# Attention sums of two neighbouring chunks issued as one stretch of array tiles

## The chip, the cores and the metric

The kernel runs on one core of one Trainium2 chip. The metric is the device time of one execution in microseconds (us), the lower the better. PE is the matrix engine (TensorE), PEld its weight loads, DVE the vector engine, ACT the scalar engine, POOL the general engine, SP the engine whose queue issues most of the DMAs. SBUF is the on-chip memory and PSUM the eight banks that matrix products are written to.

## What is computed

Three layers follow each other. The first is a linear attention with a decaying state, for 4 batches, 8 heads, 768 tokens and head dimension 48; the second a dense layer pair with a sigmoid-gated activation (3072 tokens, 384 to 2048 to 384); the third a soft mixture of 8 experts with 32 slots.

```python
for t in range(S):                                  # attention
    cur = np.einsum('bhd,bhe->bhde', u[None] * kt, vt)
    y[:, :, t] = np.einsum('bhd,bhde->bhe', rt, state + cur)
    state = wt[:, :, :, None] * state + np.einsum('bhd,bhe->bhde', kt, vt)
h = x @ w_in                                        # dense pair
x = (h * (1.0 / (1.0 + np.exp(-1.702 * h)))) @ w_out
logits = x @ phi                                    # soft experts
slot_input = softmax over tokens (logits).T @ x
out = softmax over slots (logits) @ expert outputs
```

## The kernel before

**Chunks and steps.** The tokens are cut into 24 chunks of 128 (six to a batch), and the chunks into 9 steps of 2, 2, 2, 3, 3, 3, 3, 3 and 3 chunks (`SIZES`, `BASE`). The dense pair works on a step at a time. Its hidden dimension of 2048 is cut into 16 parts, so there are 9 x 16 = 144 numbered slots `F`, with `i, f = divmod(F, 16)`. In slot F, PE issues the 9 hidden products of part F (L1272, bank `hps[F % 2]`, 256 or 384 tokens wide) and then the products of the second matrix for part F - 2 (L1407, three for each chunk of its step). ACT makes the activation (L804) and its rounded copy `gh` (L808), which waits for the second-matrix products that PE issues in the same slot, and DVE the remainder `gl` (L1111).

**The order is written out by hand.** The list `slots_of_work` says which further work stands in which slot, and each engine's program walks through the same list; each executes its own instructions strictly in this order, with semaphore waits between the engines. While step i is in the dense pair, the attention of the chunks of step i + 1 is made, in four parts `j` for each chunk (`hosts`: in a step of three chunks slots 0 to 3, 4 to 7 and 8 to 11), and behind them the expert logits of step i - 1 (`gather`).

**The attention of a chunk**, for 4 pairs `p` of heads (`par` is the head of a pair, rows 0 to 47 or 64 to 111) and its two halves `c` of 64 tokens:
- DVE scans the decays forward (`decays`, L915) and backward (`invert`, L934 and L938), makes the decayed r (`decayed`, `rp`, L944), the grown keys (`grown_keys`, `kd`, L949) and the bonus products `ruk` (L922). These are made for chunk n + 1 in the slots of chunk n, as `front_part`.
- j = 0: PE makes the scores (L1205, banks `zps`, `yps`), and turns the keys (L1306, bank `mps`), which ACT copies to `kn` (L761); DVE masks the scores (L974).
- j = 1: PE sums the bonus over each head (L1427, L1429, into `mps`), DVE multiplies it by v into `ybuf` (`bonus_values`, L985, counted by `uv_done`).
- j = 2: PE makes the state sums (L1216: keys times values of each half, into `zps` and `yps`), DVE the states `midway`, `grown` and `state` (L994, L1000, L1007).
- j = 3: PE makes the outputs (`output`, L1225 from the states, L1231 from the masked scores, into `zps` and `yps`), DVE adds them to `ybuf` (L1017). SP stores it to a scratch tensor, and loads it again as `x` in the layout of the dense pair; ACT and DVE split it (`splits`, L417, L503).

Scores, state sums and outputs are products of 48 or 64 rows by 48 or 64 columns. They run in quarters of the array: the quarter is given by the half of the rows that is read and the half of the rows that is written. The output products from the states read and write the same half, so they use two of the four quarters; the others use all four. One product of float32 operands is two records in the trace. All of `mps` is shared: key turns, bonus sums, turns of x (L1481), logits (L1494) and others are written there in turn, and before each PE waits for the reader of the last one (`mps_read`).

**Weights.** The two weight matrices are cut into quarters, eight pieces in all, that ACT rounds (`high_at`, L741) and DVE subtracts (`low_at`, L1083) in slots of step 0; the hidden products of F = 4, 8 and 12 and the second-matrix products of parts 0, 4, 8 and 12 wait for theirs.

## Time and profile before

| what | value |
|---|---|
| median of 3 runs | 606.02 us (605.09 to 606.83) |
| the profiled execution's own time | 606.68 us |
| its span in the trace | 605.0 us |
| PE busy | 585.8 us, 97% |
| DVE busy | 327.2 us, 54% |
| ACT busy | 266.3 us, 44% |
| mean granted clock of PE | 0.99 of full speed |

The span runs from the first to the last instruction; 1.7 us of the execution's own time lie outside it. Busy times count a stretch in which at least one instruction of the engine runs. In a timeline, PE's instructions overlap: the distance between two starts, and not the duration of one, says what an instruction costs.

### The profile page before, as it was taken

The page shows a single profiled execution, that of the slowest core. Times are in us where ns is not written, and L with a number is a line of the kernel's source. Part 1 is how long each engine was busy: PE and PEld are TensorE (multiplying, and loading weights), DVE is VectorE, ACT ScalarE, POOL GpSimd, SP SyncE. Part 2 cuts the span into 40 slices and gives each one's busy share as a digit, 9 for nine tenths or more (in the row PEclk, how much of TensorE's full clock was granted, in tenths as well). Part 3 has the DMA queues.
Part 4 walks back from the last instruction along what each step waited for, and adds up shares of the span by engine and source line. Part 5 has one row for each costly group of instructions (what it writes and reads, how often), then busy time and mean ns, then how long its engine had stood idle before and what let it go on. Part 6 is the DMA issues. An engine that isn't in the chain of part 4 may idle for free.

```text
span 605.0 us, 15121 instructions
## 1 busy us (share of the span) xinstructions
PE 585.8 (97%) x6335; PEld 525.4 (87%) x6335; DVE 327.2 (54%) x713; ACT 266.3 (44%) x540; POOL 10.4 (2%) x28
## 2 busy tenths in 40 slices
PE   7889899999999999999999999999999999999984
PEld 6779899899899999999999999999999999998434
DVE  8788766368565644665267535664456323323304
ACT  3955444544543344333533354335433346564313
POOL 4010000000000000000000000000000000000000
PEclk9999999999999999999999999999999999999996
DMA  8995523134322330333023312323031097668627
GB/s 282 381 259 159 158 62 97 46 88 117 102 62 79 72 94 1 102 101 89 16 76 89 101 41 63 88 65 91 2 102 27 16 366 272 212 214 302 222 97 312
DMA packets 45301, 77.50 MB, mean 128 GB/s; under 512 B 3296, under 2 KB 32480, under 8 KB 42656
## 3 DMA queue, kind: packets, MB, share of 16 engines
q1 hardware_dynamic: 44432, 73.37, 39.0%
q0 software_dynamic: 800, 3.15, 1.6%
q8 instruction: 51, 0.84, 0.6%
q14 instruction: 18, 0.15, 0.1%
HBM read 67.46 MB, written 9.04 MB: 126 GB/s over the span
## 4 chain that ended last, share of the span: by engine, by line
PE 89%; DMA 4%; DVE 4%; issue 1%; ACT 1%; SPq 0%; DVEq 0%; ACTq 0%
PE hps L1272 33%; PE acc L1407 32%; PE yps L1225 2%; DMA w2s<-w 2%; PE mps L1306 2%; PE zps L1205 2%; PE zps L1216 2%; PE mps L1481 2%; PE zps L1225 2%; DMA raw<-dmaj 1%; PE zps L1231 1%; PE mps L1494 1%; PE mps L1514 1%; PE hps L1558 1%; PE acc L1527 1%
## 5 line engine op out<-in xcount | busy, mean ns | idle before, releaser
L1111 DVE TENSOR_TENSOR gl<-g,gh 128x384 fp32r<-128x384 f32 (+1 forms) x144 | 73.9, 513 | 227.6 <-ACT gh L808 227.4
L1272 PE MATMUL hps<-xh,wi_hi 128*128 128x384 f32 (+1 forms) x432 | 147.2, 341 | 3.3 <-ACT g L804 1.7
L1272 PE MATMUL hps<-xh,wi_lo 128*128 128x384 f32 (+1 forms) x432 | 137.0, 317 | 0.0
L1272 PE MATMUL hps<-xl,wi_hi 128*128 128x384 f32 (+1 forms) x432 | 136.9, 317 | 0.0
L1407 PE MATMUL acc<-wo_hi,gh 128*128 128x384 f32 x384 | 129.3, 337 | 0.3 <-ACT x L815 0.3
L1407 PE MATMUL acc<-wo_hi,gl 128*128 128x384 f32 x384 | 129.2, 337 | 0.0
L1407 PE MATMUL acc<-wo_lo,gh 128*128 128x384 f32 x384 | 129.2, 337 | 0.0
L808 ACT ACTIVATE gh<-g 128x384 fp32r<-128x384 f32 (+1 forms) x144 | 70.4, 489 | 130.1 <-PE acc L1407 129.7
L804 ACT ACTIVATE g<-hps 128x384 f32<-128x384 f32 (+1 forms) x144 | 65.5, 455 | 130.0 <-PE hps L1272 129.7
L1272 PEld LDWEIGHTS hps<-xh,wi_hi 128*128 128x128 f32 x432 | 81.1, 188 | 13.4 <-issue 6.6
L1272 PEld LDWEIGHTS hps<-xl,wi_hi 128*128 128x128 f32 x432 | 81.5, 189 | 0.9
L1272 PEld LDWEIGHTS hps<-xh,wi_lo 128*128 128x128 f32 x432 | 81.2, 188 | 0.0
L1407 PEld LDWEIGHTS acc<-wo_hi,gh 128*128 128x128 f32 x384 | 72.1, 188 | 1.4 <-issue 0.6
L1407 PEld LDWEIGHTS acc<-wo_lo,gh 128*128 128x128 f32 x384 | 72.2, 188 | 0.0
L1407 PEld LDWEIGHTS acc<-wo_hi,gl 128*128 128x128 f32 x384 | 72.1, 188 | 0.0
L938 DVE TENSOR_TENSOR_SCAN inv<-raw,ends 112x516 f32<-112x516 f32 x24 | 29.6, 1233 | 0.8
L915 DVE TENSOR_TENSOR_SCAN decay<-raw,restart 112x516 f32<-112x516 f32 x24 | 29.4, 1225 | 1.1 <-DMA raw<-dmaj 1.1
L1225 PEld LDWEIGHTS yps<-rp,midway 48*48 48x48 f32 x384 | 22.8, 120 | 6.3 <-issue 5.5
L1225 PE MATMUL yps<-rp,midway 48*48 48x64 f32 x384 | 26.3, 218 | 0.5 <-DVE midway L994 0.5
L1225 PE MATMUL zps<-rp,state 48*48 48x64 f32 x384 | 26.0, 218 | 0.0
L922 DVE SCALAR_TENSOR_TENSOR ruk<-raw,ucols 112x128 f32<-112x128 f32 x80 | 23.6, 336 | 0.0
L1225 PEld LDWEIGHTS zps<-rp,state 48*48 48x48 f32 x384 | 22.4, 120 | 0.0
(239 smaller groups left out, 729.5 us busy)
## 6 DMA issues: line engine op xcount, KB each, us to landing
raw<-dmaj SPq DMA_DIRECT2D x23, 903.0 KB, 5.6
w1s<-w SPq DMA_DIRECT2D x16, 768.0 KB, 6.6
w2s<-w SPq DMA_DIRECT2D x16, 768.0 KB, 6.3
vn<-vnat SPq DMA_DIRECT2D x24, 192.0 KB, 2.5
tests<-wall SPq DMA_DIRECT2D x6, 768.0 KB, 15.4
out<-obuf SPq DMA_DIRECT2D x12, 384.0 KB, 3.9
y_scratch<-ybuf SPq DMA_DIRECT2D x44, 96.0 KB, 2.0
x<-y_scratch SPq DMA_DIRECT2D x22, 192.0 KB, 2.5
```

What stands on the lines that cost most here:

```text
L804: act.activation(g32[F % 2][:, 0:wide], hps[F % 2][:, 0:wide], ACT.Gelu_apprx_sigmoid).then_inc(gelu_done, 1)
L808: act.activation(gh[F % 2][:, 0:wide], g32[F % 2][:, 0:wide], ACT.Copy).then_inc(gh_done, 1)
L915: dve.tensor_tensor_scan(flat[0], flat[1], flat[2], 1.0, ALU.mult, ALU.max).then_inc(scanned, 1)
L922: last = dve.scalar_tensor_tensor(ruk[n % 2][:, p, :], field(n, RR)[:, p], ucols[:, p:p + 1], field(n, KK)[:, p], ALU.mult, ALU.mult)
L938: dve.tensor_tensor_scan(flat[0][:, ::-1], later, flat[1][:, ::-1], 1.0, ALU.mult, ALU.add).then_inc(inverted, 1)
L1111: dve.tensor_tensor(out=gl[F % 2][:, 0:wide], in0=g32[F % 2][:, 0:wide], in1=gh[F % 2][:, 0:wide].bitcast(fp32), op=ALU.subtract).then_inc ...
L1205: last = pe.matmul(score_banks(n)[par][cols, p * HALF:(p + 1) * HALF], kd[n % 2][rows, p, cols], rp[n % 2][rows, p, cols], start=True, sto ...
L1216: last = pe.matmul((zps, yps)[c][HALF * par:HALF * par + D, p * D:(p + 1) * D], kn[n % 2][rows, p, HALF * par:HALF * par + D], vn[n % 2][r ...
L1225: return pe.matmul((zps, yps)[c][rows, p * HALF:(p + 1) * HALF], (state[n % 2], midway)[c][rows, p, :], rp[n % 2][rows, p, HALF * c:HALF * ...
L1272: last = pe.matmul(hps[F % 2][:, 0:wide], w[:, g, at:at + 128], v[i % 2][:, g, 0:wide], start=m == 0, stop=m == 3 * G - 1)
L1306: last = pe.transpose(mps[:, p * R:(p + 1) * R], kd[n % 2][:, p, :], ident[0:R, 0:R])
L1407: last = pe.matmul(acc[m][:, 0:DM], a[k][:, rows], w[:, f % CW, :], start=f == 0 and w is hi and a is gh, stop=f == NF - 1 and a is gl)
```

## The change

The scores of chunk n, its state sums and the outputs of the chunk before it, o, are issued as one stretch, `meet(o, n)`. The scores move to the upper half of `zps` and `yps`, the state sums to `mps`. In the stretch PE issues the scores of n, the outputs of o from its masked scores, then a mixed part in which an output product from the state, a state sum, an output product and a state sum take turns over the four quarters, then the rest of the output products from the state, and the rest of the state sums. Two waits on PE's own products stand in it: for `crossed` before the rest of the output products, for `half_summed` before the rest of the state sums. The key turns have a slot of their own ahead of it, and the parts that DVE makes for a chunk each a slot from `part_at`. Turns of x stand a slot earlier (f = 2, 6, 10) than before, alone. Two weight pieces are subtracted a slot later on DVE, and the splits of step 1's x move from slots 10 and 15 to 11 and 14. In a step of three chunks the stretches stand at f = 3, 7 and 11, the key turns at 0, 5 and 9, the bonus sums at 4, 8 and 15.

```diff
+        part_at = {}
+
+        def place_parts(n, **slots):
+
+            for what, F in slots.items():
+                assert (F, what) not in part_at
+                part_at[F, what] = n
+
+        place_parts(2, scan=1, invert=1, grow=2, decayed=3, bonus_a=4, turn=4, bonus=6)
+        place_parts(3, scan=5, invert=6, grow=6, turn=7, decayed=7, bonus_a=8, bonus=9)
+        place_parts(4, scan=13, invert=14, grow=15, turn=16, decayed=16, bonus_a=16, bonus_b=17, split=18, bonus=19)
+        place_parts(5, scan=18, invert=19, grow=19, turn=20, decayed=20, bonus_a=20, bonus_b=21, split=22, bonus=23)
+        place_parts(6, scan=22, invert=23, grow=23, turn=24, decayed=25, bonus_a=24, bonus_b=25, split=26, bonus=27)
+        meeting_at = {5: (None, 2), 8: (2, 3), 10: (3, None), 17: (None, 4), 21: (4, 5), 26: (5, 6)}
+        for i in range(2, NST - 1):
+            n, f = BASE[i + 1] + 1, NF * i
+            place_parts(n, scan=f - 2, invert=f - 1, grow=f - 1, turn=f, bonus_a=f, bonus_b=f + 1, decayed=f + 1,
+                        split=f + 2, bonus=f + 4)
+            place_parts(n + 1, scan=f + 3, invert=f + 4, grow=f + 4, turn=f + 5, bonus_a=f + 5, bonus_b=f + 5, decayed=f + 6,
+                        split=f + 6, bonus=f + 8)
+            meeting_at[f + 3], meeting_at[f + 7], meeting_at[f + 11] = (n - 1, n), (n, n + 1), (n + 1, None)
+            if i + 1 < NST - 1:
+                place_parts(n + 2, scan=f + 7, invert=f + 8, grow=f + 8, turn=f + 9, bonus_a=f + 10, bonus_b=f + 12, decayed=f + 9,
+                            split=f + 13, bonus=f + 15)
+                meeting_at[f + 11] = (n + 1, n + 2)
+        met_in = {pair[1]: k + 1 for k, (F, pair) in enumerate(sorted(meeting_at.items()))}
+        met_out = {pair[0]: k + 1 for k, (F, pair) in enumerate(sorted(meeting_at.items()))}
...
-        hosts = {2: ((1, 2, 4, 5), (6, 8, 9, 10)), 3: ((0, 1, 2, 3), (4, 5, 6, 7), (8, 9, 10, 11))}
         splits = {2: {9: 0, 14: 1}, 3: {6: 0, 10: 1, 14: 2}}
         for i in range(NST):
-            hosted = {}
-            if i + 1 < NST:
-                chunks = hosts[SIZES[i + 1]] if i else ((4, 5, 6, 7), (8, 9, 10, 11))
-                hosted = {f: (BASE[i + 1] + m, j) for m, at in enumerate(chunks) for j, f in enumerate(at)}
+            turns = {2: "turn0", 6: "turn1", 10: "turn2"} if i < NST - 1 else {3: "turn0", 7: "turn1", 11: "turn2"}
             for f in range(NF):
-                gather = {3: "turn0", 7: "turn1", 11: "turn2", 12: "logits", 13: "turn_e", 14: "add"}.get(f)
+                gather = {**turns, 12: "logits", 13: "turn_e", 14: "add"}.get(f)
                 if i == 0 or (gather == "turn2" and SIZES[i - 1] < 3):
                     gather = None
-                slots_of_work.append((NF * i + f, hosted.get(f), (i - 1, gather) if gather else None,
-                                      soft.get(f) if i == NST - 1 else None))
-        alone = {1: (2, 0), 2: (2, 1), 3: (2, 2, 3), 13: (4, 0), 14: (4, 1), 16: (4, 2, 3)}
+                slots_of_work.append((NF * i + f, (i - 1, gather) if gather else None, soft.get(f) if i == NST - 1 else None))
         high_at = {3: 3, 5: 4, 7: 5, 9: 6, 11: 7}
-        low_at = {0: 2, 4: 3, 6: 4, 8: 5, 10: 6, 12: 7}
-        slots_of_work += [(NF * NST + f, None, None, None) for f in range(2)]
-        slots_of_work += [(None, None, (NST - 1, g), None)
+        low_at = {0: 2, 4: 3, 7: 4, 9: 5, 10: 6, 12: 7}
...
-            m = splits[SIZES[i + 1]].get(f) if i else {10: 0, 15: 1}.get(f)
+            m = splits[SIZES[i + 1]].get(f) if i else {11: 0, 14: 1}.get(f)
...
-            return (hps[0], hps[1]) if n < PRE else (zps, yps)
+            return [ps[:, 0:HP * HALF] for ps in hps] if n < PRE else [ps[:, HP * HALF:] for ps in (zps, yps)]
+
+        def sum_banks(n):
+
+            if n < PRE:
+                return zps[0:R, 0:HP * D], yps[0:R, 0:HP * D]
+            return mps[0:R, 0:HP * D], mps[0:R, HP * D:2 * HP * D]
...
+                if n >= 2 * PRE:
+                    act.wait_ge(meetings, met_in[n - 2])
+                elif n >= PRE:
...
+                if (F, "split") in part_at:
+                    n = part_at[F, "split"]
+                    act.wait_ge(ruk_made, n + 1)
+                    act.wait_ge(u_done, n)
+                    act.activation(rukh[:, :, :], ruk[n % 2][:, :, :], ACT.Copy).then_inc(rukh_done, 1)
+                if (F, "turn") in part_at:
...
-                if n >= 2:
-                    dve.wait_ge(av_done, n - 1)
...
+                if n >= 2 * PRE:
+                    dve.wait_ge(meetings, met_out[n - 2])
+                elif n >= PRE:
+                    dve.wait_ge(av_done, n - 1)
+                dve.tensor_tensor(out=rp[n % 2][:, :, :], in0=field(n, RR), in1=decay[n % 2][:, :, 0:C],
+                                  op=ALU.mult).then_inc(decayed_done, 1)
 
...
+                if (F, "scan") in part_at:
+                    decays(part_at[F, "scan"])
+                if (F, "invert") in part_at:
+                    invert(part_at[F, "invert"])
+                if (F, "grow") in part_at:
+                    grown_keys(part_at[F, "grow"])
+                if (F, "decayed") in part_at:
+                    decayed(part_at[F, "decayed"])
+                if (F, "bonus_a") in part_at:
+                    n = part_at[F, "bonus_a"]
+                    if n < FULL:
+                        products(n)
+                    else:
+                        bonus(n, 0)
+                if (F, "bonus_b") in part_at:
+                    bonus(part_at[F, "bonus_b"], 1)
+                if (F, "split") in part_at:
+                    n = part_at[F, "split"]
+                    dve.wait_ge(rukh_done, n - FULL + 1)
+                    dve.wait_ge(u_done, n)
+                    dve.tensor_tensor(out=rukl[:, :, :], in0=ruk[n % 2][:, :, :], in1=rukh[:, :, :].bitcast(fp32),
+                                      op=ALU.subtract).then_inc(rukl_done, 1)
+                if F in low_at:
+                    low_part(low_at[F])
+                if F in meeting_at:
+                    before, n = meeting_at[F]
+                    if before is not None:
+                        add_output(before)
+                    if n is not None:
+                        first_state(n)
                         mask_scores(n)
-                        if n >= FULL:
-                            dve.wait_ge(rukh_done, n - FULL + 1)
-                            dve.wait_ge(u_done, n)
-                            dve.tensor_tensor(out=rukl[:, :, :], in0=ruk[n % 2][:, :, :], in1=rukh[:, :, :].bitcast(fp32),
-                                              op=ALU.subtract).then_inc(rukl_done, 1)
...
+                if (F, "bonus") in part_at:
+                    bonus_values(part_at[F, "bonus"])
...
+            def meet(o, n):
+
+                both = n is not None and (n + 1) % CB
+
+                def score_tile(par, c, p):
+                    rows, cols = slice(HALF * par, HALF * par + D), slice(HALF * c, HALF * (c + 1))
+                    return pe.matmul(score_banks(n)[par][cols, p * HALF:(p + 1) * HALF], kd[n % 2][rows, p, cols],
+                                     rp[n % 2][rows, p, cols], start=p == 0, stop=o is None, skip_group_check=True)
+
+                def from_block(c, par, p):
+                    h = 2 * p + par
+                    rows = slice(HALF * c, HALF * (c + 1))
+                    return pe.matmul((zps, yps)[c][HALF * par:HALF * par + D, p * HALF:(p + 1) * HALF],
+                                     vn[o % 2][rows, h * D:(h + 1) * D], scores[rows, par, p, :],
+                                     start=False, stop=False, skip_group_check=True)
+
+                def from_state(c, par, p):
+                    rows = slice(HALF * par, HALF * par + D)
+                    return pe.matmul((zps, yps)[c][rows, p * HALF:(p + 1) * HALF], (state[o % 2], midway)[c][rows, p, :],
+                                     rp[o % 2][rows, p, HALF * c:HALF * (c + 1)], start=False, stop=c != par, skip_group_check=True)
+
+                def sum_tile(c, par, p, first):
+                    h = 2 * p + par
+                    rows = slice(HALF * c, HALF * (c + 1))
+                    return pe.matmul(sum_banks(n)[c][HALF * par:HALF * par + D, p * D:(p + 1) * D],
+                                     kn[n % 2][rows, p, HALF * par:HALF * par + D], vn[n % 2][rows, h * D:(h + 1) * D],
+                                     start=first and p == 0, stop=True, skip_group_check=True)
+
+                for p in range(HP):
+                    for c in range(2):
+                        for par in range(2):
+                            score_tile(par, c, p)
+                if o is not None:
+                    for p in range(HP):
+                        for c in range(2):
+                            for par in range(2):
+                                last = from_block(c, par, p)
+                    last.then_inc(crossed, 1)
+                for p in range(HP):
+                    if o is not None:
+                        from_state(0, 0, p)
+                    last = sum_tile(0, 1, p, True)
+                    if o is not None:
+                        from_state(1, 1, p)
+                    if both:
+                        last = sum_tile(1, 0, p, True)
+                last.then_inc(half_summed, 1)
+                if o is not None:
+                    pe.wait_ge(crossed, o + 1)
+                    for p in range(HP):
+                        for par in range(2):
+                            from_state(1 - par, par, p)
+                pe.wait_ge(half_summed, n - PRE + 1)
+                for p in range(HP):
+                    last = sum_tile(0, 0, p, not both)
+                    if both:
+                        last = sum_tile(1, 1, p, False)
+                last.then_inc(meetings, 1)
...
+                if (F, "turn") in part_at:
+                    n = part_at[F, "turn"]
+                    pe.wait_ge(*mps_read)
+                    pe.wait_ge(front, n + 1)
+                    turn_keys(n)
+                    mps_read = (kn_done, n + 1)
+                if F in meeting_at:
+                    o, n = meeting_at[F]
+                    pe.wait_ge(y_done, n if o is None else o)
+                    if n is None:
+                        outputs(o)
+                    else:
+                        if o is not None:
+                            pe.wait_ge(midway_done, o + 1)
+                            if (o + 1) % CB:
+                                pe.wait_ge(grown_done, growths(o))
+                        pe.wait_ge(scored, 2 * n)
                         pe.wait_ge(*mps_read)
-                    if j == 0:
-                        turn_keys(n)
-                        mps_read = (kn_done, n + 1)
-                    if j == 1 and n < FULL:
+                        pe.wait_ge(decayed_done, n + 1)
+                        pe.wait_ge(kn_done, n + 1)
+                        pe.wait_ge(vn_in[n % 2], 16 * (n // 2 + 1))
+                        meet(o, n)
+                        mps_read = (grown_done, growths(n)) if (n + 1) % CB else (midway_done, n + 1)
+                if (F, "bonus") in part_at:
...
+                if (F, "bonus") in part_at:
+                    n = part_at[F, "bonus"]
+                    pe.wait_ge(*mps_read)
+                    if n < FULL:
                         bonus_sums(n)
...
-                        mps_read = (uv_done, n + 1)
```

Where lines are left out, the waits of ACT and DVE on a chunk's products become waits on the count of finished stretches (`meetings`, with `met_in` and `met_out`), `first_state` reads the sums from `sum_banks`, `output` takes its semaphore as an argument, and the loops lose the entry `attn`.

## Rows read from the trace of the kernel before

**Rows 1.** The page: busy time by engine.

```profile
PE 585.8 (97%) x6335; PEld 525.4 (87%) x6335; DVE 327.2 (54%) x713; ACT 266.3 (44%) x540; POOL 10.4 (2%) x28
```

**Rows 2.** Waits of PE: engine line <- releaser: us, times, longest.

```profile
PE hps L1272 <- DVE xl L503: 1.6, 1, 1.6
...
PE zps L1205 <- DVE kd L949: 0.8, 1, 0.8
```

**Rows 3.** Busy time by stretch: us, PE, PEld, DVE, ACT, POOL, clock, DMA, GB/s.

```profile
30.00:75.09 45.09, 41.02 (x512) 38.39 (x510) 37.06 (x63) 23.23 (x43) 3.17 (x4) 1.00 0.69 195
...
140.00:490.00 350.00, 350.00 (x3926) 323.93 (x3925) 190.44 (x426) 145.34 (x303) 0.00 (x0) 1.00 0.26 74
```

**Rows 4.** Timeline of PE, scores and key turns: start us, us, what.

```profile
252.46 0.34 PE L1407 MATMUL acc<-wo_hi,gl 128*128 128x384 f32 x1
252.73 0.27 PE L1205 MATMUL zps<-rp,kd 48*64 48x64 f32 x1
...
253.20 0.22 PE L1205 MATMUL zps<-rp,kd 48*64 48x64 f32 x1
...
253.35 0.60 PE L1306 MATMUL mps<-ident,kd 112*128 112x112 f32 x4
...
253.99 0.34 PE L1272 MATMUL hps<-xl,wi_hi 128*128 128x384 f32 x1
```

**Rows 5.** Timeline of PE, bonus sums (256.94), then state sums (260.65).

```profile
256.94 0.39 PE L1427 MATMUL mps<-rukh,headsum 112*112 112x512 f32 x1
...
257.40 0.34 PE L1272 MATMUL hps<-xh,wi_hi 128*128 128x384 f32 x1
...
260.38 0.34 PE L1407 MATMUL acc<-wo_hi,gl 128*128 128x384 f32 x1
260.65 0.25 PE L1216 MATMUL zps<-vn,kn 64*48 64x48 f32 x2
...
261.43 0.34 PE L1272 MATMUL hps<-xl,wi_hi 128*128 128x384 f32 x1
```

**Rows 6.** Timeline of PE, outputs of a chunk and the turn of x.

```profile
264.22 0.34 PE L1407 MATMUL acc<-wo_hi,gl 128*128 128x384 f32 x1
264.49 0.25 PE L1225 MATMUL yps<-rp,midway 48*48 48x64 f32 x1
...
265.31 0.25 PE L1231 MATMUL zps<-scores,vn 64*48 64x64 f32 x1
...
265.82 0.22 PE L1231 MATMUL yps<-scores,vn 64*48 64x64 f32 x1
...
266.53 0.34 PE L1272 MATMUL hps<-xl,wi_hi 128*128 128x384 f32 x1
```

**Rows 7.** Timeline of PE, a bonus and the next slot, 256 tokens wide.

```profile
82.84 0.39 PE L1427 MATMUL mps<-rukh,headsum 112*112 112x512 f32 x1
...
85.38 0.49 PE L1481 MATMUL mps<-ident,x 128*128 128x128 f32 x3
...
85.82 0.28 PE L1272 MATMUL hps<-xl,wi_hi 128*128 128x256 f32 x1
```

**Rows 8.** Timeline of DVE in a slot with a bonus, and grown keys.

```profile
257.76 0.56 DVE L1111 TENSOR_TENSOR gl<-g,gh 128x384 fp32r<-128x384 f32 x1 [0.83 <-ACT gh L808]
258.23 0.68 DVE L985 TENSOR_TENSOR ybuf<-mps,raw 112x512 f32<-112x512 f32 x1
258.83 0.17 DVE L934 RECIPROCAL ends<-decay 112x4 f32<-112x4 f32 x1
259.04 1.23 DVE L938 TENSOR_TENSOR_SCAN inv<-raw,ends 112x516 f32<-112x516 f32 x1
...
265.69 0.68 DVE L949 TENSOR_TENSOR kd<-raw,inv 112x512 f32<-112x512 f32 x1
```

**Rows 9.** Timelines: DVE, a weight quarter subtracted; PE, start of F = 8.

```profile
49.72 1.75 DVE L1083 TENSOR_TENSOR wi_lo<-stage,wi_hi 128x1536 fp32r<-128x1536 f32 x1
...
52.08 0.39 PE L1272 MATMUL hps<-xh,wi_hi 128*128 128x256 f32 x1
```

103 lines of the change are left out of this document (32 added, 71 removed).

## Prediction

> **What bounds the kernel now.** I read the page first, then PE's waits, the stretches, and last the timelines. PE is busy 97% of the span [rows 1], and its waits after the start-up are few: 0.8 us for grown keys at F = 4 and 1.6 us for a split of x at F = 16 [rows 2]. From 140 to 490 us it has no idle time at full clock, and DVE is busy 190 of 350 us; before 75 us DVE is the fuller engine, 37.1 of 45.1 us [rows 3]. So time can be won only by giving PE less to issue, and is lost wherever PE is made to wait. The reader should see two things in the timelines: what a block of small products costs between two wide ones, and how late DVE finishes in a slot.
>
> A block's cost is the distance from the last wide product ahead of it to the second one behind it, less two wide products of 0.174 us. Scores and key turns: 253.99 - 252.46 - 0.35 = 1.18 us, of which the turns are 0.37 (253.35 to the next wide product at 253.72) [rows 4]. Bonus: 257.40 - 256.94 = 0.46. State sums: 261.43 - 260.38 - 0.35 = 0.70 [rows 5]. Outputs with a turn of x: 1.96, outputs alone 1.68 (found so in the six blocks without it), so the turn adds 0.28 [rows 6]. Chunks 2 to 23 repeat this within 0.02 us, but for the waits named.
>
> **Merging the blocks.** Inside a block the array is paced by its fullest quarter. Scores start at 252.73 and their last group of four quarters at 253.20 [rows 4]: 0.060 us a group, 8 groups, 0.5 us. Output products from the state use two quarters and take 16 groups in 265.31 - 264.49 = 0.82 and a little more that overlaps, 0.9 us; those from the scores 0.45 [rows 6]. The state sums' 8 groups are 0.36, which is their 0.70 less entry and exit. So entering and leaving cost about 0.34 us in each block (0.70 - 0.36; 1.68 - 1.34; 0.81 - 0.48).
>
> The mixed part takes no load off the fullest quarter: a quarter that reads and writes the same half did 20 products of a chunk before (4 scores, 4 sums, 12 for outputs) and does 20 after. Estimate of a stretch: scores 0.50, outputs from scores 0.45, mixed part 0.46 (paced by the output products), rest of the outputs 0.45, rest of the sums 0.36 (only two quarters, but as many groups), entry and exit 0.28: 2.50 us. The two new waits on PE's own products each have some 0.45 us of other work ahead of them, and one product lasts 0.22 [rows 6]; I cost them at nothing. If that cover failed they would cost up to 0.3 us each. In the two stretches without an old chunk the second wait is bare: 1.74 us instead.
>
> Before, scores, sums and outputs were (1.18 - 0.37) + 0.70 + 1.68 = 3.19 us a chunk; key turns alone will be 0.40 instead of 0.37, and a turn of x alone 0.32 (85.82 - 85.38 - 0.12 [rows 7]) instead of 0.28. For chunks 4 to 23: before 20 x 3.56 = 71.2; after 20 x 0.40 + 1.74 + 19 x 2.50 + 1.68 = 58.9, and 16 x 0.05 for x. **Gain 11.5 us**, bounds 5 (both waits bare in half the stretches) and 14 (no loss by turns, entry as low as a full-size product's).
>
> **The wait it adds.** In the new order a bonus block of chunk n and the key turns of chunk n + 1 stand in neighbouring slots, f + 4 and f + 5, f + 8 and f + 9, f + 15 and f + 16. Both are written to `mps`, so the turns wait for `uv_done`, that is for DVE's `bonus_values`; and in the bonus slot DVE has, in this order, the split `gl`, the backward scan, the grown keys, and only then `bonus_values`. Count from the moment PE starts the bonus, 256.94. `gl` starts 0.82 later; the next instruction follows at +0.48, so the reciprocal is at 1.30; the scan 0.21 later, 1.51; it lasts 1.23, to 2.74; the grown keys wait for its result and start at 2.78; `bonus_values`, which has the same size, follows 0.60 behind (258.83 - 258.23), 3.38, and ends 0.68 later at 4.06 [rows 8]. PE can go on at about 4.12. PE itself arrives after 0.46 for the bonus and 18 wide products: the next block's place is at 260.38 + 0.17 = 260.55, which is 3.61 [rows 5]. **PE stands still for 0.51 us**, with its whole queue behind it, in each turn of chunks 11 to 23: 13 x 0.5 = 6.5 us. Before, the next user of `mps` behind a bonus came two slots later, and grown keys had a slot to themselves.
>
> While steps 1 and 2 pass, slots are 256 tokens wide and PE arrives sooner: 85.38 - 82.84 = 2.54 us after the bonus [rows 7]. DVE is little faster (copy and split of 256 tokens save about 0.24 in all, an estimate by size from 0.56 [rows 8]), 3.88. Turns of chunks 5, 6, 8 and 9 wait 1.34 each; that of chunk 7, with no bonus ahead but the grown keys in the slot just before, (3.88 - 0.60) = 3.28 - 2.08 = 1.2; of chunk 10, in a slot partly wide, 0.8. Together 7.3 us. A stall does not pile up: it ends before DVE's next split is wanted. Bounds for all 19: 0.25 us less each (9 us in all) and 0.25 more (18.5). I take **13.8 us lost**.
>
> **Step 0.** The subtraction of weight piece 4 stands at F = 7, and the hidden products of F = 8 need it. Following DVE's order: F = 6 has `gl`, backward scan, grown keys, `bonus_values`; F = 7 has `gl`, the decayed r, then the piece of 1.75 us. From F = 6's `gl` that is 0.35 + 1.4 + 0.65 + 0.65 + 0.35 + 0.6 + 1.7, 5.7 us, against some 3 us in which PE makes the products of F = 7. By my walk the piece ends at 53.9 us instead of 51.5 and F = 8 begins at 53.9 instead of 52.1 [rows 9], with the outputs of chunk 2 still to come. Behind it the pieces at F = 9 and 12 hold the second-matrix products of F = 10 and 14 for 0.7 us each (POOL's two last loads also start later, since they wait for pieces 4 and 5), and a wait of some 0.8 for the split of x at F = 16 stays of 1.6; the 0.8 us for keys at F = 4 goes. Sum: F = 16 begins **3.3 us later**, bounds 0 and 6, since each of these waits is the difference of two long sums.
>
> **Moves that cost nothing.** SP loads chunk n + 2's raw fields after `uv_done` of n, now nearly a slot earlier in a step than the scan needs by some 2 us (landing takes less than the two to three slots between); stores of y still start at f = 3, 7, 11, directly behind the stretch, and reach the splits at 6, 10, 14 with over 2 us to spare. If either cover went, a late load would show as a DVE wait ahead of a scan or an ACT wait ahead of a split. DVE's work in the slot behind a stretch (2.4 us for outputs, states and masks) ends ahead of its next `gl`. `bonus_b` at f = 12 delays the expert maximum by 0.5 us, and PE reads it a slot later. The tail is unchanged.
>
> **Sum.** - 11.5 + 13.8 + 3.3 = + 5.6 us. On the profiled execution (span 605.0 and 1.7 outside it, 606.7) that is 612.3; the median shown is 0.7 below that execution, so I forecast 611.6.
>
> **A rule that speaks against the stretch.** Before, quarters that read the upper and the lower rows at the same time never wrote to one bank: the state sums of the first half went to `zps`, of the second to `yps` [rows 5]. Now both go to `mps`, in different partitions. No row shows that case. If such pairs ran one behind the other, the rest of the sums would take 0.72 instead of 0.36, and the mixed part 0.72 (two sums of 0.045 a group in series) instead of 0.46: 0.62 x 22 = 13.6 us more, 625 us. The Trainium skill, "TensorEngine Tiling (Array Packing)", section "Gotcha 1: PSUM Pressure", says that different row tiles cannot access one PSUM bank at the same time, and leaves the care to the software; by that rule this rival would hold, or sums would be wrong.
>
> **The rivals.**
> 1. The new waits don't form, because DVE is ahead of my count or the parts are shorter: 606.0 - 11.5 + 3.3 = 598 us. For it: DVE is idle half the time over the long stretch [rows 3]. Against: the idle time lies ahead of `gl`, whose start PE itself sets [rows 8]. 0.11.
> 2. Waits about half as long and nothing lost in step 0: 606.0 - 11.5 + 8 to 11, 603 to 606. The place is the same `mps` wait. 0.10.
> 3. Row halves in one bank serialise: 625 us. 0.07.
> 4. The change does not do what it says: mixed products don't overlap, and each group takes 0.058 + 0.045. 8 x 0.045 x 21 = 7.6 us more, 619 us. 0.06.
> The forecast, slower by the wait for `bonus_values`, has 0.66; the decisive point is 3.61 against 4.12 us after a bonus begins, and the sign of the whole turns if DVE finishes 0.3 us sooner.
>
> **How the numbers follow.** About 0.3% (1.8 us) is what a measurement can tell from no change. Slower: 0.66 + 0.07 + 0.06 = 0.79; within 0.3%: most of rival 2, 0.08; faster: rival 1 and the rest of 2, 0.13. The forecast's own range is 608 to 615.5; the range reaches down to 606 and up to 618, which leaves out rivals 1, 3 and the tops of the others, 2 in 10.
>
> **What would show it.** Right: PE waits on DVE `ybuf` (`bonus_values`) ahead of key turns, about 19 times, near 0.5 us in wide steps and over 1 us before 240 us; key turns alone 0.40; a stretch of 2.5 us; F = 8 beginning near 54 us, behind a weight piece. Wrong: PE idle under 3 us in all between 80 and 500 us, or a stretch over 2.9 us.

## The result, and the profile after

The changed kernel takes 622.43 us (median of 4 runs, 621.31 to 624.44) where the kernel before takes 605.85 us in the runs beside it: a ratio of 1.0277, 95% interval 1.0245 to 1.0308. It is slower, as forecast, but by 16.6 us instead of 5.6, and 622.4 lies above the range of 606.0 to 618.0. The profiled execution took 621.96 us with a span of 620.2, which is 15.2 us longer than the span before.

The page of the changed kernel: its span and busy times [rows 1].

```profile
span 620.2 us, 15141 instructions
PE 582.7 (94%) x6335; PEld 524.6 (85%) x6335; DVE 332.2 (54%) x713; ACT 262.9 (42%) x540; POOL 10.6 (2%) x28
```

PE has 3.1 us less of busy time, but its share fell from 97% to 94%: the time went into waits. PE's waits of the changed kernel (us in total, times, longest), which answer to [rows 2]:

```profile
PE mps L1402 <- DVE ybuf L1008: 8.8, 19, 1.2
PE hps L1368 <- ACT g L837: 3.1, 2, 1.6
PE acc L1503 <- DVE wo_lo L1112: 2.2, 2, 1.4
PE hps L1368 <- DVE wi_lo L1112: 2.0, 1, 2.0
PE acc L1503 <- ACT x L848: 2.0, 6, 0.4
...
PE mps L1402 <- DVE kd L984: 1.1, 1, 1.1
PE mps L1538 <- DVE rukl L1162: 0.8, 2, 0.4
```

L1402 are the key turns, L1368 the hidden products, L1503 those of the second matrix, L1538 the bonus. The first row is the wait the prediction was built on. That it counts 19, the number forecast, is in part chance: one of them, 0.8 us, is that of chunk 3 at F = 7, which the prediction didn't count, and the wait of chunk 7, which it did count, is the row for `kd`, whose keys it had named as the cause. The next four rows were not foreseen, or only in part. This list counts a wait from the modelled end of the product before, about 0.2 us behind the point at which the next product could have gone (products come every 0.174 us but are shown 0.34 long), so distances between products, used below, give somewhat more.

Stretches of the changed kernel: us, then busy time of PE, PEld, DVE, ACT and POOL, granted clock, DMA share, GB/s. They answer to [rows 3].

```profile
30.00:83.16 53.16, 44.62 (x508) 41.49 (x508) 35.97 (x58) 22.63 (x43) 3.17 (x4) 0.94 0.58 165
50.00:53.30 3.30, 0.60 (x4) 0.39 (x4) 3.26 (x5) 2.33 (x3) 0.00 (x0) 1.00 0.47 138
54.00:57.00 3.00, 3.00 (x13) 2.75 (x11) 0.00 (x0) 0.38 (x1) 0.30 (x1) 0.50 0.84 274
76.00:80.00 4.00, 2.63 (x13) 2.46 (x12) 3.42 (x4) 0.90 (x3) 0.00 (x0) 0.69 0.11 36
```

Step 0, up to the first hidden product of F = 16, ends at 83.18 us instead of 75.09. PE stands from 50 to 53.3 us, all but 0.6, and then runs at half the clock (1.2 of 2.4 GHz) from 54 to 57 us; a second fall, also of 3.4 us, follows at 77.6 us (0.69 is the mean of that stretch). The kernel before had the clock at 1.00 in this stretch [rows 3]. Counting from the first hidden product of F = 0 (30.24 before, 29.90 after) to F = 16 and on to F = 143 (546.58 and 562.29), the difference falls apart so:

```
                        before    after    difference   forecast
F = 0 to F = 16          44.85    53.28      +8.4         +3.3
F = 16 to F = 143       471.49   479.11      +7.6         +2.3
```

The merged stretch itself came out as worked out. PE's timeline of the changed kernel, second half of a merged stretch; it answers to [rows 4], [rows 5] and [rows 6]:

```profile
280.24 0.27 PE L1291 MATMUL zps<-rp,kd 48*64 48x64 f32 x1
...
280.76 0.22 PE L1297 MATMUL zps<-scores,vn 64*48 64x64 f32 x1
...
281.20 0.22 PE L1303 MATMUL zps<-rp,state 48*48 48x64 f32 x1
281.21 0.21 PE L1309 MATMUL mps<-vn,kn 64*48 64x48 f32 x2
281.23 0.22 PE L1303 MATMUL yps<-rp,midway 48*48 48x64 f32 x1
...
282.10 0.54 PE L1309 MATMUL mps<-vn,kn 64*48 64x48 f32 x16
282.57 0.45 PE L1368 MATMUL hps<-xh,wi_hi 128*128 128x384 f32 x1
```

Scores take 0.52 us, outputs from scores 0.44, the mixed part with the rest of the outputs 0.90, the rest of the sums 0.47 with the exit. By the prediction's measure (distance less two wide products) the stretch costs 2.51 to 2.53 us in 19 of 20 cases, and 2.7 in the one at F = 8, where the wide product ahead of it still ran at half the clock; 1.82 without an old chunk, 1.68 for outputs alone, 0.41 for key turns that don't wait, 0.33 for a turn of x.

The wait, in DVE's timeline of the changed kernel, which answers to [rows 8], and in PE's with it:

```profile
269.80 0.56 DVE L1140 TENSOR_TENSOR gl<-g,gh 128x384 fp32r<-128x384 f32 x1 [1.62 <-ACT gh L841]
270.27 0.18 DVE L964 RECIPROCAL ends<-decay 112x4 f32<-112x4 f32 x1
270.48 1.23 DVE L968 TENSOR_TENSOR_SCAN inv<-raw,ends 112x516 f32<-112x516 f32 x1
271.75 0.69 DVE L984 TENSOR_TENSOR kd<-raw,inv 112x512 f32<-112x512 f32 x1
272.36 0.68 DVE L1008 TENSOR_TENSOR ybuf<-mps,raw 112x512 f32<-112x512 f32 x1
```

```profile
268.98 0.39 PE L1538 MATMUL mps<-rukh,headsum 112*112 112x512 f32 x1
...
272.42 0.34 PE L1503 MATMUL acc<-wo_hi,gl 128*128 128x384 f32 x1
273.10 0.60 PE L1402 MATMUL mps<-ident,kd 112*128 112x112 f32 x4 [0.34 <-DVE ybuf L1008]
```

The bonus starts at 268.98. PE arrives at the turns at 272.59, 3.61 us later, and starts them at 273.10, 4.12 us later: both as the prediction counted.

### The profile page after: what moved, and what is told of

It is laid out like the page before. It is cut to its first block, busy times and chain, and to the rows that moved or that the text cites. A ratio compares the mean times of both kernels' runs of the same rounds, so it can differ in the third digit from the quotient of the medians.

```text
span 620.2 us, 15141 instructions
## 1 busy us (share of the span) xinstructions
PE 582.7 (94%) x6335; PEld 524.6 (85%) x6335; DVE 332.2 (54%) x713; ACT 262.9 (42%) x540; POOL 10.6 (2%) x28
## 4 chain that ended last, share of the span: by engine, by line
PE 73%; DVE 9%; issue 6%; DMA 6%; ACT 4%; SPq 2%; POOL 0%; ACTq 0%; DVEq 0%; POOLq 0%
PE acc L1503 27%; PE hps L1368 26%; DVE inv L968 4%; DMA spare<-w_in 3%; DVE ybuf L1008 2%; PE mps L1402 2%; ACT gh L841 2%; PE zps L1291 2%; PE mps L1309 2%; DVE gl L1140 2%; PE yps L1303 1%; DMA stage<-w_out 1%; PE acc L1632 1%; PE mps L1586 1%; PE mps L1619 1%
## 5 line engine op out<-in xcount | busy, mean ns | idle before, releaser
L1368 PE MATMUL hps<-xh,wi_hi 128*128 128x384 f32 (+1 forms) x432 | 147.5, 341 | 5.5 <-ACT g L837 3.1
L1368 PE MATMUL hps<-xl,wi_hi 128*128 128x384 f32 (+1 forms) x432 | 137.6, 318 | 0.4 <-issue 0.4
L1368 PE MATMUL hps<-xh,wi_lo 128*128 128x384 f32 (+1 forms) x432 | 137.6, 319 | 0.0
L1503 PE MATMUL acc<-wo_hi,gh 128*128 128x384 f32 x384 | 130.5, 340 | 4.2 <-DVE wo_lo L1112 2.2
L1503 PE MATMUL acc<-wo_lo,gh 128*128 128x384 f32 x384 | 130.0, 339 | 0.0
L1503 PE MATMUL acc<-wo_hi,gl 128*128 128x384 f32 x384 | 129.9, 338 | 0.0
L1368 PEld LDWEIGHTS hps<-xh,wi_hi 128*128 128x128 f32 x432 | 81.7, 189 | 15.9 <-issue 6.0
L1368 PEld LDWEIGHTS hps<-xl,wi_hi 128*128 128x128 f32 x432 | 82.0, 190 | 1.5 <-issue 0.6
L1368 PEld LDWEIGHTS hps<-xh,wi_lo 128*128 128x128 f32 x432 | 81.7, 189 | 0.0
L1503 PEld LDWEIGHTS acc<-wo_hi,gh 128*128 128x128 f32 x384 | 72.7, 189 | 6.6 <-DVE gl L1140 4.0
L1503 PEld LDWEIGHTS acc<-wo_lo,gh 128*128 128x128 f32 x384 | 72.8, 190 | 0.0
L1503 PEld LDWEIGHTS acc<-wo_hi,gl 128*128 128x128 f32 x384 | 72.7, 189 | 0.0
L1402 PE MATMUL mps<-ident,kd 112*128 112x112 f32 x96 | 14.3, 271 | 9.9 <-DVE ybuf L1008 8.8
L1309 PE MATMUL mps<-vn,kn 64*48 64x48 f32 x640 | 23.4, 205 | 0.1
L1402 PEld LDWEIGHTS mps<-ident,kd 112*128 112x128 f32 x96 | 9.6, 140 | 16.4 <-DVE ybuf L1008 14.8
L1303 PE MATMUL zps<-rp,state 48*48 48x64 f32 x320 | 21.5, 216 | 0.0
```

The lines of the kernel that those rows point to most:

```text
L1303: return pe.matmul((zps, yps)[c][rows, p * HALF:(p + 1) * HALF], (state[o % 2], midway)[c][rows, p, :], rp[o % 2][rows, p, HALF * c:HALF * ...
L1309: return pe.matmul(sum_banks(n)[c][HALF * par:HALF * par + D, p * D:(p + 1) * D], kn[n % 2][rows, p, HALF * par:HALF * par + D], vn[n % 2] ...
L1368: last = pe.matmul(hps[F % 2][:, 0:wide], w[:, g, at:at + 128], v[i % 2][:, g, 0:wide], start=m == 0, stop=m == 3 * G - 1)
L1402: last = pe.transpose(mps[:, p * R:(p + 1) * R], kd[n % 2][:, p, :], ident[0:R, 0:R])
L1503: last = pe.matmul(acc[m][:, 0:DM], a[k][:, rows], w[:, f % CW, :], start=f == 0 and w is hi and a is gh, stop=f == NF - 1 and a is gl)
```

## The experiments

My theory after the result had two halves. In the steady steps, PE waits for `bonus_values`, which stands behind 1.4 us of scan work on DVE in the same slot. In step 0, weight pieces come late, PE stands still, and the clock falls behind it. The rivals: DVE is simply full, so that work put elsewhere brings the wait back there; or the merged stretch itself costs more than it saves. All edits are made to the changed kernel. The experiments were measured in several sets, and the medians of the kernel before in them lie between 605.7 and 606.7 us, so a difference of under 1 us between two sets says nothing. What is read from a trace is read from one execution.

**1. Scans and growth one slot earlier**, from chunk 7 on.

```
- place_parts(n, scan=f - 2, invert=f - 1, grow=f - 1, turn=f, ...
+ place_parts(n, scan=f - 3, invert=f - 3, grow=f - 2, turn=f, ...
- place_parts(n + 1, scan=f + 3, invert=f + 4, grow=f + 4, ...
+ place_parts(n + 1, scan=f + 2, invert=f + 3, grow=f + 3, ...
- place_parts(n + 2, scan=f + 7, invert=f + 8, grow=f + 8, ...
+ place_parts(n + 2, scan=f + 7, invert=f + 7, grow=f + 7, ...
```

> The changed kernel with the backward scan and the grown keys one slot earlier than the bonus of the chunk before, from chunk 7 on, nothing else. Theory (the turn of the keys waits because grown keys and bonus_values stand in one DVE slot): the 13 waits of 0.55 us before key turns in wide steps and those of chunks 7 to 10 (1.3, 1.4, 1.4 and 0.4) go, 11 us, less up to 2 for outputs that DVE adds later: 611 to 613 us. Rival (DVE simply has too much to do between two turns, the wait comes back in another place, before a stretch or a bonus): 619 to 623 us, with new PE waits of 0.5 us behind DVE.

Measured: 617.60 us (614.74 to 619.19), ratio 1.0169 (1.0132 to 1.0206). PE's waits of this kernel:

```profile
PE mps L1538 <- DVE gathered L1228: 1.9, 1, 1.9
PE mps L1402 <- DVE ybuf L1008: 1.8, 3, 0.8
```

And a stretch of it:

```profile
185.30:188.70 3.40, 3.40 (x12) 3.31 (x11) 0.69 (x1) 0.01 (x1) 0.00 (x0) 0.50 0.33 85
```

The waits for `bonus_values` fell from 19 to 3 and from 8.8 to 1.8 us, and all key turns from chunk 7 on cost 0.40. But F = 16 to F = 143 shrank only by 4.9 us (474.2 from 479.1), since the bonus, now behind the grown keys and the scan, waited instead: 1.9 us once at 184.9 us, for work that DVE had not yet come to, and by less in eight other slots, 2.6 us in all by distances; the split of x at F = 32 came 0.8 us late. Right behind the wait of 1.9 us the clock stood at 0.50 for 3.4 us, and slot 48 took 1.4 us longer for it. The total lies between the theory's 611 to 613 and the rival's 619 to 623. The place of the wait is shown; so is half of the rival. Moving DVE's work into the slot of other work brings the wait along.

**2. Only the key turns of a stretch's first chunk one slot later.**

```
- place_parts(n, scan=f - 2, invert=f - 1, grow=f - 1, turn=f, ...
+ place_parts(n, scan=f - 2, invert=f - 1, grow=f - 1, turn=f + 1, ...
```

> The changed kernel with the key turn of the first chunk of each later step at f = 1 instead of f = 0 (6 turns). Theory: this removes the wait of 0.55 us before 5 of these turns and of 1.3 and 0.4 before those of chunks 7 and 10, and gives back the cover of 0.4 us between the copies of x on ACT and the second-matrix products of f = 2, whose 6 waits of 0.35 go too: 2.2 + 1.7 + 2.0 = 6 us, 616 us. Rival (the copies of x wait on something else than the missing work in slot f = 1): only 4 us, and the 0.35 us waits stay.

Measured: 616.35 us (615.40 to 617.05), ratio 1.0155 (1.0134 to 1.0176). PE's waits:

```profile
PE mps L1402 <- DVE ybuf L1008: 7.2, 14, 1.2
```

F = 16 to F = 143 took 472.9 us, 6.2 less. Six key turns fell to 0.40 us, and of the six waits of `acc L1503` for ACT's copy of x (2.0 us together in the list of the changed kernel) one is left: the turn now stands in the slot in which ACT makes that copy, and covers it. Before, PE's bonus stood there. The one that is left, at F = 130, is in the kernel before as well (0.32 us at 502.4 us). So five are new, 1.6 us in that list, a term that the prediction has nowhere.

**3. The stretch cut once.** One 128-column product on the whole array is put between the scores and the outputs from scores in each merged stretch. It adds work and changes no value that is read.

```
+ pe.matmul(mps[:, 384:512], warm[:, 0:128], warm[:, 128:256], start=True, stop=True)
```

> The changed kernel with one full-array product of 128 columns put between the scores and the outputs in each of the 20 stretches that have both. Theory (entering and leaving the quarters costs 0.34 us in each block, and the merger won 2 x 0.34 a chunk): each stretch grows by 0.3 to 0.45 us (0.34, and 0.05 to 0.1 for the product), 2.53 to about 2.9, 7 us in all, 629 us. Rival (the gain of the merger came from elsewhere, mode changes are free): 2.6 us a stretch, 623 to 624 us.

Measured: 631.84 us (628.63 to 633.22), ratio 1.0403 (1.0365 to 1.0441). The stretch went from 2.53 to 2.93 us, 0.40 more, in 17 of 20; the other three are longer still, one behind a fall of the clock. The total grew by 9.4 us, where 7 were forecast: 20 x 0.40 is 8.0, and in the profiled execution the clock also fell once more, from 34.7 to 38.1 us, behind PE's wait at F = 2. A 128-column product is 0.06 us by the 0.174 of one of 384, so one more passage from small tiles to the whole array and back costs about 0.34, the figure the prediction took from [rows 5] and [rows 6]. The Trainium skill, "TensorEngine Tiling (Array Packing)", section "Key Properties", says that changing the tiling mode drains TensorE; the trace agrees in that each passage costs time, and can't tell how much of the 0.34 is the drain. So the merger saves what it was meant to save, and the rival that the stretch costs more than it earns falls.

**4. The array kept busy before F = 8.** Twelve 128-column products into `hps[0]`, which nobody reads, while PE waits for the weight piece.

```
+ if F == 8:
+     pe.wait_ge(gelu_done, F - 1)
+     for _ in range(12):
+         pe.matmul(hps[0][:, 0:128], ident[:, :], ident[:, :], start=True, stop=True)
```

> The changed kernel with 12 products of 128 columns on PE while it waits for weight piece 4 ahead of the hidden products of F = 8. Theory (the standstill of 3 us let the granted clock fall to 1.2 GHz, and the products of F = 8 ran at half speed for 3.5 us): the products of F = 8 stand 0.12 and 0.17 us apart instead of 0.21 and 0.32, F = 9 starts 1.6 us sooner (near 57.9 instead of 59.5), and the end comes 1 to 2 us sooner if DVE does not take it back. Rival (they are slow because the weights were just written or the DMA is busy): spacing stays 0.21 and 0.32.

Measured, a single run: 619.9 us, span 618.2. Stretches of this kernel, to be read beside the same three of the changed kernel above:

```profile
50.00:53.30 3.30, 3.02 (x27) 3.02 (x28) 2.83 (x4) 1.95 (x3) 0.18 (x1) 1.00 0.69 173
54.00:57.00 3.00, 3.00 (x108) 2.75 (x108) 0.80 (x2) 0.80 (x2) 0.00 (x0) 1.00 0.95 295
76.00:80.00 4.00, 3.47 (x13) 3.50 (x14) 2.49 (x6) 0.83 (x2) 0.00 (x0) 0.57 0.00 0
```

F = 8 starts as late as in the changed kernel (53.33), but its products run at full clock, and F = 9 starts at 57.92 instead of 59.49. In the changed kernel the fall of the clock there cost 1.6 us, on top of the standstill. The second fall stays, from 76.5 us on. This is one execution of each, and experiments 5 and 7 show the clock staying up at this place without any such products; so it is shown what half the clock costs, and not that the twelve products kept it up.

**5. Weight piece 5 one slot earlier.**

```
- low_at = {0: 2, 4: 3, 7: 4, 9: 5, 10: 6, 12: 7}
+ low_at = {0: 2, 4: 3, 7: 4, 8: 5, 10: 6, 12: 7}
```

> The changed kernel with weight piece 5 subtracted at F = 8, as before the change, instead of F = 9; piece 4 stays at F = 7. Theory (the chain over step 0: piece 5 releases the last weight load of POOL, which now leaves 7 us late and lands at 73 us, then ACT rounds piece 7 before its activation of F = 12, and PE waits for it at F = 14): the last load leaves near 60.5 instead of 64.8, the wait of 0.9 us at F = 10 goes and that of 1.5 us at F = 14 shrinks below 0.5; F = 16 starts 2 to 4 us sooner, 618 to 620 us. Rival (the step is bound by DVE's amount of work, not by this piece's place): F = 16 starts less than 1 us sooner, 621 to 623 us.

Measured: 616.79 us (615.98 to 617.34), ratio 1.0187 (1.0170 to 1.0204). F = 9 to F = 16 took 18.8 us, where the changed kernel took 23.7 and the kernel before 19.7. That one piece was the late one: POOL's last load waits for it, was issued at 59.3 us instead of 64.8, and landed 5.1 us later; both waits at F = 14 and the one at F = 10 are gone. F = 16 starts 6.4 us sooner, more than the 2 to 4 of the theory. Two stretches of this kernel show why:

```profile
50.00:53.30 3.30, 0.60 (x4) 0.39 (x4) 3.30 (x5) 2.32 (x3) 0.00 (x0) 1.00 0.47 120
54.00:57.00 3.00, 3.00 (x106) 2.75 (x107) 0.74 (x2) 0.80 (x2) 0.34 (x1) 1.00 0.92 273
```

PE stood just as long (0.60 of 3.30 us busy), and the clock did not fall, nor did it later in step 0. Those two falls cost the changed kernel some 2.8 us (below), so about 3.6 us are the piece's.

Experiment 7 shows the same again, and better: its program is that of the changed kernel up to slot 34.

```profile
50.00:53.30 3.30, 0.73 (x5) 0.52 (x6) 3.12 (x4) 2.19 (x3) 0.00 (x0) 1.00 0.55 143
54.00:57.00 3.00, 3.00 (x113) 2.75 (x113) 0.93 (x2) 0.80 (x2) 0.15 (x1) 1.00 0.91 286
```

The same standstill, of 2.00 us in PE's waits ahead of F = 8 and 0.76 to 0.82 ahead of the key turns before it, stands in seven of the traces. In five (the changed kernel, experiments 1, 2, 3 and 6) the clock stood at 0.50 behind it, in two (5 and 7) it stayed at 1.00. The same idle time can be followed by half the clock or not.

**6. The raw fields kept from meeting the last weight load.** SP waits before it loads the fields of chunk 5.

```
+ if n == 3:
+     sp.wait_ge(stage_in[1], 32)
```

> The changed kernel with SP holding back the raw fields of chunk 5 until the last weight piece has landed. Theory (its landing took 8.4 us because the raw fields of 0.9 MB were issued 0.3 us behind it): it lands in 5.5 to 6 us, ACT rounds piece 7 near 70.7 instead of 73.2, the waits at F = 14 and of its second-matrix products shrink by 1.5 to 2.5 us in all, and F = 16 starts 1.5 to 3 us sooner. Rival (the landing was slow for another reason, such as POOL's issue): no change over 0.5 us at F = 16.

Measured, a single run: 623.0 us. First ACT's timeline of the changed kernel, then of this one:

```profile
73.20 1.48 ACT L772 ACTIVATE wo_hi<-stage 128x1536 fp32r<-128x1536 f32 x1 [3.00 <-DMA stage<-w_out]
```

```profile
71.33 1.49 ACT L774 ACTIVATE wo_hi<-stage 128x1536 fp32r<-128x1536 f32 x1
```

In the changed kernel the load is issued at 64.80 and ACT can use it at 73.20, 8.4 us; the raw fields are issued 0.3 us behind it. Here it is issued at 65.8 and used 5.5 us later. So with the raw fields issued beside it the load takes some 3 us longer. But everything behind SP's wait came late too, the store of y and the load of x, and PE's waits show where it ended:

```profile
PE hps L1370 <- DVE xl L534: 2.7, 1, 2.7
```

F = 9 to F = 16 gained 1.8 us; F = 16 starts 0.8 us sooner, between the rival's 0.5 and the theory's 1.5 to 3, and the total gained nothing. Two falls of the clock have a part in that: the one at F = 8 lasted 6.8 us in this execution instead of 3.4, and F = 9 began 1.0 us later; and behind the wait for `xl` the clock stood at 0.50 from 83.2 to 86.6 us, where F = 16 took 4.0 us instead of 2.5. The mend is an earlier load, as in 5, not a wait on SP.

**7. The backward scan into DVE's gap.** DVE is idle between the stretch's own work and the next `gl`; the scan goes there, in the slot of the forward scan, and the growth stays.

```
- place_parts(n + 1, scan=f + 3, invert=f + 4, grow=f + 4, ...
+ place_parts(n + 1, scan=f + 3, invert_late=f + 3, grow=f + 4, ...
- place_parts(n + 2, scan=f + 7, invert=f + 8, grow=f + 8, ...
+ place_parts(n + 2, scan=f + 7, invert_late=f + 7, grow=f + 8, ...
+ if (F, "invert_late") in part_at:
+     invert(part_at[F, "invert_late"])
```

> The changed kernel; from chunk 7 on the backward scan with its reciprocal of the second and third chunk of a stretch is put behind the stretch's own VectorE work one slot earlier (in the slot of the forward scan), and no longer ahead of bonus_values in the slot of the key turns. The growth and the rest stay where they are. Theory (key turns wait because bonus_values ends behind 1.4 us of scan work, and VectorE idles some 1.5 us behind the stretch's work in the slot before): the nine waits of about 0.55 us before wide key turns go, and most of those of chunks 8 and 9, together 7 to 8 us, with nothing in their place: 614 to 615 us of 622.4, and step 2 to the end about 7 us shorter. Rival (VectorE is full there too, as when scan and growth both came a slot earlier): half comes back as waits for grown or xl, 618 to 619 us.

Measured: 615.14 us (614.53 to 616.39), ratio 1.0158 (1.0143 to 1.0172). DVE's timeline of this kernel, and its wait row:

```profile
264.14 0.35 DVE L1033 TENSOR_TENSOR state<-grown,decay 112x192 f32<-112x192 f32 x1
264.41 0.17 DVE L964 RECIPROCAL ends<-decay 112x4 f32<-112x4 f32 x1
264.62 1.23 DVE L968 TENSOR_TENSOR_SCAN inv<-raw,ends 112x516 f32<-112x516 f32 x1
266.12 0.56 DVE L1140 TENSOR_TENSOR gl<-g,gh 128x384 fp32r<-128x384 f32 x1 [0.26 <-ACT gh L841]
266.59 0.68 DVE L984 TENSOR_TENSOR kd<-raw,inv 112x512 f32<-112x512 f32 x1
267.19 0.68 DVE L1008 TENSOR_TENSOR ybuf<-mps,raw 112x512 f32<-112x512 f32 x1
```

```profile
PE mps L1404 <- DVE ybuf L1008: 3.9, 9, 0.8
```

The scan ends 0.26 us before the next split wants DVE, and no wait comes in its place. F = 16 to F = 143 is 472.3 us, 6.9 less. The four wide waits that stay (at 249, 314, 378 and 443 us) belong to the first chunks, which experiment 2 treats. The total is at the theory's 614 to 615 and not at the rival's 618 to 619. Against experiment 1 this tells the two theories apart: DVE is not full. What counts is what stands between the split and `bonus_values`.

**8. Step 0 laid out anew.**

```
- place_parts(3, scan=5, invert=6, grow=6, turn=7, decayed=7, bonus_a=8, bonus=9)
+ place_parts(3, scan=5, invert=6, grow=7, turn=8, decayed=8, bonus_a=8, bonus=10)
- meeting_at = {5: (None, 2), 8: (2, 3), 10: (3, None), ...
+ meeting_at = {5: (None, 2), 9: (2, 3), 11: (3, None), ...
- low_at = {0: 2, 4: 3, 7: 4, 9: 5, 10: 6, 12: 7}
+ low_at = {0: 2, 4: 3, 6: 4, 8: 5, 10: 6, 12: 7}
- m = splits[SIZES[i + 1]].get(f) if i else {11: 0, 14: 1}.get(f)
+ m = splits[SIZES[i + 1]].get(f) if i else {12: 0, 15: 1}.get(f)
```

> The changed kernel with step 0 alone laid out anew: the growth of chunk 3 in slot 7, its key turn in slot 8, the joint stretch of chunks 2 and 3 in slot 9, the outputs of chunk 3 in slot 11, the first pieces of output weights in slots 2, 3, 4, 5, 6, 7 at 0, 4, 6, 8, 10, 12, the splits of step 1 in slots 12 and 15. Theory (the excess of step 0, 8.4 us up to slot 16, is the late weight pieces and the standstill they cause, with the fall of the granted clock behind it): the standstill before slot 8 falls under 0.8 us, no stretch before slot 16 stands at half clock, slot 16 starts at 74 to 76 us instead of 83.2, and the total is 614 to 615 us. Rival (the excess is the stretch's own cost in step 0, or moves to another late piece): slot 16 at 79 us or later and 618 us or more.

Measured: 618.71 us (616.48 to 619.59), ratio 1.0215 (1.0200 to 1.0230). The profiled execution is the fastest of the four, 616.48 us: in it F = 8 starts at 51.86, F = 16 at 77.63, 5.6 us earlier than in the changed kernel, and the clock is full all through and behind step 0. The other three took 1.8 to 3.1 us longer, at a mean clock of 0.987 to 0.992 against 0.993. The standstill before F = 8 is 1.1 us, not under 0.8, F = 16 is 1.6 us behind the theory's band, and the total 4 us. The total is where the rival had it and F = 16 is not, so this lies between the theory and the rival, which had said that the excess moves to another late piece. What took the place is in the waits of this kernel:

```profile
PE hps L1368 <- ACT g L837: 2.4, 1, 2.4
PE hps L1368 <- DVE xl L534: 2.1, 1, 2.1
```

The wait for `g` is at F = 2, in the start-up, where the changed kernel has 1.6 us of it; it is 0.8 us longer in this execution. That for `xl`, before F = 16, comes because chunk 3's outputs, with which the way of x into step 1 begins, are now a slot later.

**9. All mends together**: 2, 7 and 8, and chunks 4 to 6 spread the same way.

```
- place_parts(4, scan=13, ..., bonus_b=17, split=18, bonus=19)
+ place_parts(4, scan=13, ..., bonus_b=17, split=17, bonus=19)
- place_parts(5, scan=18, invert=19, grow=19, turn=20, ..., split=22, bonus=23)
+ place_parts(5, scan=16, invert_late=17, grow=18, turn=20, ..., split=21, bonus=23)
- place_parts(6, scan=22, invert=23, grow=23, turn=24, ...
+ place_parts(6, scan=22, invert=22, grow=23, turn=24, ...
```

> The changed kernel with all the mends together: the key turns of the first chunk of a stretch one slot later, the backward scan behind the stretch's work, chunks 4 to 6 in step 1 spread in the same way, and step 0 laid out anew. Theory (the joint stretch earns the 11.5 us of the forecast, and what it loses is where the parts were put): turn later gave 6.1, the scan gives 7 to 8, step 0 gives 7 to 8, chunks 4 to 6 give 2 to 3; the sum, 622.4 less 22 to 25, is 597 to 601 us, under the 605.8 of the kernel before. Rival (gains overlap, or the waits come back elsewhere): 603 to 608 us, no better than before.

Measured: 602.60 us (600.79 to 603.18, 6 runs), ratio 0.9939 (0.9926 to 0.9952): 0.6% faster than the kernel before, which is little but clear of the interval, and short of the theory by 2 us, at the edge of the rival's 603 to 608. Two stretches of this kernel show the rest:

```profile
75.00:76.80 1.80, 0.00 (x0) 0.00 (x0) 1.50 (x3) 0.63 (x2) 0.00 (x0) 1.00 0.00 0
76.00:82.00 6.00, 5.20 (x29) 5.17 (x29) 1.48 (x4) 1.26 (x3) 0.00 (x0) 0.72 0.00 0
```

The standstill for `xl` from experiment 8 is there, and this time the clock falls behind it (0.72 is the mean of a stretch that ran partly at full and partly at half the clock).

**10. The outputs of chunk 3 back in slot 10**, the rest as in 9.

```
- place_parts(3, ..., bonus_a=8, bonus=10)
+ place_parts(3, ..., bonus_a=8, bonus=9)
- meeting_at = {5: (None, 2), 9: (2, 3), 11: (3, None), ...
+ meeting_at = {5: (None, 2), 9: (2, 3), 10: (3, None), ...
- m = splits[SIZES[i + 1]].get(f) if i else {12: 0, 15: 1}.get(f)
+ m = splits[SIZES[i + 1]].get(f) if i else {12: 0, 14: 1}.get(f)
```

> The kernel with all the mends together, but with the outputs of chunk 3 one slot earlier (slot 10 instead of 11, its bonus in slot 9, the split for step 1 in slot 14 instead of 15). In the trace of that kernel TensorE stands 2.1 us before slot 16, for the x of step 1 whose way (y store, x load, xh, xl) begins with those outputs at 67.0 us, and the granted clock falls to 0.67 to 0.77 right behind, where slots 17 and 18 take 4.5 and 2.4 us against 3.9 and 2.5 and more. Theory: x then comes 2 us earlier, the standstill falls under 0.8 us, no stretch from 76 to 82 us is under full clock, and the total falls by 2 to 4 us, to 599 to 601 us of 602.6. Rival (the standstill moves to the low half of the last weights, or to kd, in slots 10 to 15): 602 us or more.

Measured: 599.82 us (599.17 to 599.89, 4 runs), ratio 0.9896 (0.9880 to 0.9913). The waits and a stretch of this kernel:

```profile
PE mps L1411 <- DVE grown L1026: 1.5, 1, 1.5
PE hps L1370 <- ACT g L837: 1.5, 1, 1.5
PE hps L1370 <- DVE wi_lo L1112: 1.4, 1, 1.4
...
PE hps L1370 <- DVE xl L534: 0.7, 1, 0.7
```

```profile
76.00:82.00 6.00, 5.44 (x70) 5.11 (x72) 4.12 (x9) 2.76 (x8) 0.00 (x0) 1.00 0.00 0
```

The wait for `xl` is 0.7 us and the clock stays at 1.00. (The expectation gave the slots behind the fall with wrong numbers; F = 16 took 4.07 us in experiment 9 and 2.50 here, so the fall cost 1.6.) The standstill moved in part to slot 9, where chunk 3's bonus now waits 1.5 us for the grown keys behind the stretch, much as the rival had it; but F = 16 starts at 76.01. From F = 32 to F = 143, where nothing of step 0 or 1 is left, this kernel takes 417.0 us, the kernel before 426.7 and the changed kernel 430.3. With most of its waits gone the merger is worth 9.7 us there. Whether the kernel before would gain from step 0's new places by themselves was not tried.

## Why the prediction was wrong in size

The prediction had the cause of the loss, the sign, and two of its three terms right. Two steps failed, and each is about half of the miss: the term for step 0, 3.3 us where the runs showed 8.4, and, from F = 16 on, moves that were taken as free, where the sum had + 2.3 us and the runs showed + 7.6.

**The merger: right.** Forecast 2.50 us a stretch, 1.74 without an old chunk, 0.40 for key turns; measured 2.53, 1.82 and 0.41. Chunks 4 to 23: 20 x 0.41 + 1.82 + 19 x 2.53 + 1.68 = 59.8 against 71.2 before and forecast 58.9. The two waits on PE's own products cost nothing beyond that. Experiments 3 and 10 confirm it from both sides.

**The wait for `bonus_values`: right.** Forecast 13.8 us. Measured by distances, 13 wide turns cost 0.96 instead of 0.41 (0.55 each, 7.2 us; forecast 6.5), chunks 5 to 10 lose 0.72, 0.75, 1.28, 1.38, 1.39 and 0.42 (5.9 us; forecast 7.3): 13.1 us. Chunks 5 and 6 lose half of the 1.34 forecast; the bonus ahead of each was itself held up, by 0.66 and 0.64 us (below), and the two together come to 1.4, which fits. Experiments 1, 2 and 7 take the wait away piece by piece.

**Step 0: failed.** "Bounds 0 and 6, since each of these waits is the difference of two long sums": it was 8.4 us. The late piece was as said: it ends at 53.26 instead of the forecast 53.9, and F = 8 starts at 53.31. The 3.3 doesn't follow from the terms that are named with it: 1.8 for F = 8, 0.7 and 0.7, less 0.8 for x, are 2.4; the outputs of chunk 2, "still to come", have no price. Two things were left out or put too low.
- The clock. PE's standstill ahead of F = 8 was followed by half the clock: 1.6 us (experiment 4), and some 1.2 us more at the second fall, by F = 14 to F = 16 in the changed kernel and experiment 5, less their waits. The term has nothing for it. The trace of before had the clock at 1.00 in all of step 0, but it did show such a fall, in its tail, which the prediction doesn't use. Two stretches of the kernel before:

```profile
586.00:589.50 3.50, 1.81 (x14) 0.37 (x6) 0.53 (x1) 0.98 (x2) 0.00 (x0) 1.00 0.00 0
590.00:596.00 6.00, 6.00 (x20) 6.00 (x20) 4.71 (x9) 4.24 (x9) 0.00 (x0) 0.50 0.66 258
```

- The last weight load. The prediction put POOL's two last loads "also later", and then priced the pieces behind them at 0.7 us each. The last load was issued at 64.80 instead of 58.04, met the raw fields of chunk 5 and took 8.4 us; ACT stood 3.0 us for it, and behind that PE 1.5 us for `g` and 1.4 for the low half at F = 14. Together 2.9 where the term had 0.7.

By distances in the two traces: F = 8 came 1.6 us later; the blocks of F = 8 to F = 15 are 0.7 longer, with the outputs of chunk 2 among them; the wait at F = 10 cost 1.1 and the two at F = 14 3.2; the wait for x at F = 16 is 1.2 shorter; the two falls cost 1.6 and 1.2. That is 8.2 of the 8.4. Experiment 5 takes 6.4 us of it back by one slot's shift of one piece, part of it because the clock did not fall in that execution. How much of the median each fall is, is not shown, since it differs from run to run: the mean clock of the four runs of the changed kernel is 0.983 to 0.989, of experiment 5 0.988 to 0.995.

**"Moves that cost nothing": two that it doesn't name did cost.** The bonus left slot f + 1, where it had covered ACT's copy of x: five new waits, 1.6 us, gone in experiment 2. And the bonus of chunks 4, 5 and 9 now comes before its low half or the gathered sums: 1.13, 1.11 and 0.88 us instead of 0.47, 1.7 us. So from F = 16 on: + 13.1 + 1.6 + 1.7, and 0.8 for turns of x alone, less 11.4 for the merger, makes 5.8 of the 7.6 measured. One longer `add` is 0.3, and 0.7 a standstill in slot 40, at 160 us, for which the trace names nobody; 0.8 stays unassigned. The kernel before has no such standstill; of the ten experiments' traces eight have one in the same slot and one has it in the slot before. Its cause stays open.

**The rivals.** 1 (no new waits, 598) and 2 (half waits) are refuted by the 13.1 us. 4 (mixed products don't overlap) would show each group of the mixed part at 0.10 us; from 281.20 to 282.10 there are 16 groups of output products, the sums beside them, at 0.056 a group. 3 (halves in one bank serialise, 625) came nearest to the measured time by number alone and is false by its mechanism: both row halves' sums go to `mps` at 282.10, eight products in 16 records that the timeline merges into one line, and the next full product is at 282.57, with the exit in between, where the prediction counted 0.72 for them in series. The rule of the Trainium skill that it rested on ("TensorEngine Tiling (Array Packing)", "Gotcha 1: PSUM Pressure") does not decide the time here: the trace differs from it, at least where the two halves write different partitions of the bank.

## What to carry to other kernels

Price a standstill of the bounding engine twice: its own length, and what the clock and the queues do behind it; a late buffer release moves the next load into other traffic. When a slot loses an operation, ask what other engine's work it was covering. And before giving up a reordering for the waits that it brings, look at what stands ahead of each late result: here scans moved into an idle gap, turns moved by one slot and earlier weight pieces turned a loss of 16.6 us into a gain of 5.9 (1.0%).

## What the runs showed of the hardware that was not expected

- An idle stretch of TensorE need not lower its clock. With 0.60 of 3.30 us busy the granted clock went to 0.50 in the changed kernel and stayed at 1.00 in experiment 5, and with 0.73 busy in experiment 7, whose program is the same up to there; a wait of 2.1 us before F = 16 was followed by 0.50 for 3.4 us in experiment 9 and by 1.00 in experiment 8. The Trainium skill, "TensorE: Matmul & The Clock Gate", says in Part 1 of the slow products at the start of a kernel that their number varies from run to run of the same kernel; here the same is seen in the middle of one.
- A single wait of 1.9 us, with PE busy in the 3.0 us before it, was followed by half the clock for 3.4 us (experiment 1, at 185 us).
- A 768 KB weight load took 8.4 us to landing with 903 KB of raw fields issued 0.3 us behind it, and 5.5 us without.
- A passage from small tiles to a product on the whole array and back costs about 0.34 us in this kernel, in the middle of a stretch as at its ends (0.40 less an estimated 0.06 for the product that was put in).
